# Second chunk's values one step sooner: a regrouped ScalarE and VectorE order for its last tiles, in top-k attention fused with two feed-forward layers

## The reference

```
scores = scale * q @ k.T                              # per batch and head, 576 x 576
kth    = 32nd largest of each row
attn   = softmax(where(scores >= kth, scores, -1e9))
x      = (attn @ v) as 2304 tokens x 512
x      = max(0.01 * h, h) @ w_out    with h = x @ w_in            # layer 0: 512 -> 2048 -> 512
out    = g @ w_out2                  with h = x @ w_in2           # layer 1
         g = h where h >= 1, 0 where h <= -1, (h + 1)^2 / 4 between
```

## Time and profile before

| | before |
|---|---|
| median of 3 runs | 1165.05 us (1163.45 to 1166.36) |
| time of the profiled execution | 1163.93 us |
| its span, first to last instruction | 1162.1 us |
| TensorE matmul busy | 1092.6 us, 94% |
| VectorE busy | 877.2 us, 75% |
| ScalarE busy | 791.6 us, 68% |
| GpSimd busy | 464.8 us, 40% |
| mean granted TensorE clock | 0.979 |

### The profile page before, as it was taken

How to read it: one execution, slowest core, us unless ns; L and a number is a source line. 1 busy time by engine, 2 the same in 40 slices (tenths; PEclk the granted TensorE clock), 3 DMA queues, 4 the chain that set the end, 5 groups by cost and what they waited for, 6 DMA issues and landing times.

```text
span 1162.1 us, 21227 instructions
## 1 busy us (share of the span) xinstructions
PE 1092.6 (94%) x7568; PEld 1002.3 (86%) x7568; DVE 877.2 (75%) x1921; ACT 791.6 (68%) x1827; POOL 464.8 (40%) x493
## 2 busy tenths in 40 slices
PE   5457998899999999999999999999999999999998
PEld 3336887799988998899999879989998999999998
DVE  7999999889889998999979989888993005300234
ACT  7887999787788877887869868778885224322332
POOL 5654468552264432643225434225532234222322
PEclk9679999999999999999999999999999999999999
DMA  7988988697657788788667667565555677787764
GB/s 247 351 337 298 366 307 311 217 377 252 234 201 237 246 307 289 274 291 293 237 232 245 220 218 247 203 211 192 169 195 210 213 257 253 254 285 251 256 246 139
DMA packets 90680, 295.52 MB, mean 254 GB/s; under 512 B 10064, under 2 KB 13776, under 8 KB 90576
## 3 DMA queue, kind: packets, MB, share of 16 engines
q1 hardware_dynamic: 86544, 289.45, 71.2%
q10 hardware_dynamic: 4032, 4.72, 1.1%
HBM read 255.85 MB, written 38.27 MB: 253 GB/s over the span
## 4 chain that ended last, share of the span: by engine, by line
PE 69%; DVE 18%; ACT 5%; issue 3%; POOL 3%; DMA 1%; SPq 0%; POOLq 0%; ACTq 0%; DVEq 0%
PE ps_f L928 19%; PE ps_f L936 18%; PE ps_f L929 18%; DVE top L1211 8%; DVE work L1215 7%; PE ps_av L887 6%; PE ps_s L848 3%; PE ps_t L864 2%; DVE part_r L1238 2%; PE ps_t L870 2%; DMA raw<-wd 1%; PE ps_t L848 1%; POOL gate L741 1%; ACT probs L1056 1%; ACT probs L1048 1%
## 5 line engine op out<-in xcount | busy, mean ns | idle before, releaser
L1211 DVE MAX8 top<-work 128x8 f32<-128x576 f32 x432 | 310.2, 743 | 0.2
L928 PE MATMUL ps_f<-xy,w_ring 128*128 128x384 f32 (+2 forms) x896 | 289.3, 323 | 5.7 <-ACT gate L1115 2.0
L928 PE MATMUL ps_f<-gate,w_ring 128*128 128x384 f32 (+2 forms) x896 | 285.2, 318 | 0.0
L936 PE MATMUL ps_f<-gate,w_ring 128*128 128x384 f32 (+2 forms) x896 | 280.9, 314 | 4.1 <-POOL gate L741 4.0
L936 PE MATMUL ps_f<-xy,w_ring 128*128 128x384 f32 (+2 forms) x896 | 281.1, 314 | 1.6 <-POOL xy L751 1.1
L929 PE MATMUL ps_f<-xy,w_ring 128*128 128x384 f32 (+2 forms) x896 | 280.3, 313 | 0.0
L929 PE MATMUL ps_f<-gate,w_ring 128*128 128x384 f32 (+2 forms) x896 | 279.8, 312 | 0.0
L1215 DVE MATCH_REPLACE8 work<-top,work 128x576 f32<-128x576 f32 x288 | 213.3, 740 | 0.0
L741 POOL TENSOR_TENSOR gate<-part_r,gate 128x384 fp32r<-128x384 f32 (+2 forms) x112 | 101.3, 905 | 244.0 <-ACT gate L1115 243.9
L928 PEld LDWEIGHTS ps_f<-xy,w_ring 128*128 128x128 f32 x896 | 169.7, 189 | 19.9 <-issue 10.1
L928 PEld LDWEIGHTS ps_f<-gate,w_ring 128*128 128x128 f32 x896 | 169.2, 189 | 6.5 <-issue 6.2
(11 more groups left out here) (85 smaller groups left out, 1842.0 us busy)
## 6 DMA issues: line engine op xcount, KB each, us to landing
w_ring<-w_split SPq DMA_DIRECT2D x408, 512.0 KB, 4.2
w_split<-w_ring SPq DMA_DIRECT2D x40, 512.0 KB, 6.3
raw<-wd SPq DMA_DIRECT2D x64, 256.0 KB, 5.8
w_split<-xy SPq DMA_DIRECT2D x24, 512.0 KB, 5.0
v_sb<-vd SPq DMA_DIRECT2D x32, 320.0 KB, 5.7
kq<-kqd SPq DMA_DIRECT2D x16, 480.0 KB, 4.9
kq<-kqd SPq DMA_DIRECT2D x15, 416.0 KB, 3.6
out_t<-y_acc ACTq DMA_DIRECT2D x12, 192.0 KB, 4.3
```

Source lines behind the costliest of these rows:

```text
L928: pe.matmul(out, w[:, 0, m], high, start=first, stop=False)
L936: mm = pe.matmul(out, w[:, 0, m], low, start=False, stop=end)
L1211: op = dve.max(top[:, t % TOP_SLOTS, 8 * r:8 * r + 8], source(t, r))
```

## The change

Four things change together.

1. `out_step` of items 18 and 19 is their last tile plus 5 instead of 6: they are transposed in steps 39 and 40, not in 40 and 41. Item 17 stays at 38. The values of gp 7 follow in step 40, not 41, so `READY[1]` is 41. The planner's `FIRST_FILL` becomes 3987 ns, and by its loop units 0 to 43 lie in steps 21 to 40, unit 44 is in step 41, and every later step holds what the step after it held, within one unit; units 248 to 335 are left for step 152. The order of the units is the same.
2. In steps 36 to 39, in which no ordinary tile has its exponential, the hurried tile (32 to 35) takes the ordinary place on ScalarE: `keep` ahead of the first group, `exponential` right behind it. Items 18 and 19 are normalised on ScalarE in their own step, behind the exponential, rather than in the step before.
3. VectorE's iteration 36 is written out: it ends tile 35 (third and fourth round) and then begins tile 36, closing item 18 in between.
4. Item 19's sum is closed in the middle of VectorE's iteration 37 rather than at its end.

```diff
+def sooner(it):
+    return hurried(it.gp) and it.gp == ITEM_OF[it.first - 1].gp
+
 def out_step(it):
-    return it.last + (5 if starts_early(it.gp) else 6 if hurried(it.gp) else 7)
+    return it.last + (5 if starts_early(it.gp) or sooner(it) else 6 if hurried(it.gp) else 7)
...
+SECOND_END = LAST_OF_GROUP[CHUNKS[1].last_gp]
...
                 done, t, soon = OUT_AT.get(s), exp_tile(s), hurried_tile(s)
+                if t is None and s >= READY[0]:
+                    t, soon = soon, None
...
                 if t is not None:
                     exponential(t)
-                if s + 1 in OUT_AT:
+                if done and sooner(done):
+                    normalise(done)
+                if s + 1 in OUT_AT and not sooner(OUT_AT[s + 1]):
                     normalise(OUT_AT[s + 1])
...
+            def finish_second(t, count, shut, first, second, third):
+                dve.wait_ge(dve_step, count)
+                top8(t - 1, 2)
+                for u in first:
+                    event(u)
+                dve.wait_ge(dve_step, count + 1)
+                drop8(t - 1, 2)
+                for u in second:
+                    event(u)
+                dve.wait_ge(dve_step, count + 2)
+                top8(t - 1, 3)
+                for u in third:
+                    event(u)
+                dve.wait_ge(scores_copied, 2 * ITEM_OF[t].n + 2)
+                top8(t, 0)
+                close_sum(shut)
+                dve.wait_ge(dve_step, count + 3)
+                drop8(t, 0)
+                dve.wait_ge(dve_step, count + 4)
+                invert_sum(shut)
+                if by_dve(shut):
+                    normalise(shut)
+                dve.wait_ge(dve_step, count + 5)
+                top8(t, 1)
+                dve.wait_ge(dve_step, count + 6)
+                drop8(t, 1)
...
-                early = shut is not None and starts_early(shut.gp)
+                early = shut is not None and (starts_early(shut.gp) or shut.last == SECOND_END)
...
+                if t == SECOND_END + 1:
+                    finish_second(t, count, shut, first, second, third)
                     count += 7
                     continue
```

More of the change, by code:

```diff
@@ L1277, in _ @@
                     finish_first(t, count)
+                    count += 7
+                    continue
+                if t == SECOND_END + 1:
+                    finish_second(t, count, shut, first, second, third)
                     count += 7
```

## The result

| | before | after |
|---|---|---|
| median, five runs each | 1164.2 us (1163.45 to 1166.36) | 1158.91 us (1158.24 to 1160.18) |
| ratio | | 0.9955, 95% interval 0.9944 to 0.9967 |
| span of the profiled execution | 1162.1 us | 1157.1 us |
| TensorE matmul busy | 1092.6 us | 1093.6 us |
| mean granted clock | 0.979 | 0.984 |

The kernel became 5.3 us faster; 5.5 was forecast. (The median before is of five runs here and of three in the table ahead of the prediction, 1165.05.) That the sum came so close is luck: two of its terms were wrong, by 2.0 and 2.8 us, and their errors nearly cancelled. The windows of the changed kernel, with the same columns as the earlier trace rows, show the stretch around the edit and what lies behind it.

A forecast was written before the change was run, and what follows sets the result against it. TensorE, busy 1092.6 of 1162.1 us, bounds the kernel, so only its waits and lower clock could move. Terms 1.7 + 1.5 + 1.3 + 1.4 - 0.4 = 5.5 us gave 1158.4, or 1159.5 against the median; range 1157 to 1161.5.

The forecast's parts named there:

- The gap ahead of gp 7's values: Step 40: TensorE waits about 1.2 us in all instead of 2.89; 1.7 us gained, between nothing and 2.9.
- its clock: Values of gp 7 run at full clock once the wait shrinks to pieces under a microsecond; 1.56 us gained, or nothing.
- Item 21's scores: Their wait for item 16's copy falls from 1.76 to about 0.5: 1.3 us gained, plus 1.37 from gp 6's clock.
- The shortest wait with a low clock: Around gp 6's and gp 7's values: 1.76 us is the shortest wait a low clock follows; shorter ones left open.
- The ScalarE-paced stretch: Steps in the thirties: waits of 1.8, 1.7 and 0.96 us stay; nothing gained, between 1.5 us more and 2 less.
- Later steps: Behind the edit: 15 scores or values products with little cover before, 16 after; 0.4 us lost.
- slower by the slip: Rival, steps 41 to 151: new pairings of units and items lose 10.3 us against 5.9 won, near 1169; chance 0.10.
- VectorE's order: Iteration 36: `finish_second` costs VectorE 0.6 us through waits between scans, hidden by its own 2.92 us wait; nothing.
- The clock falls all the same: Rival: waits shrink, but the clock still falls before gp 6's and gp 7's values; gain 2.6 us, 1162.5; chance 0.08.
- The waits only move: Rival: ScalarE's lag reappears at a bank or item 16's copy; gain 0 to 3.4 us, around 1163; chance 0.18.
- Everything is won: Rival: waits of the paced stretch shrink too; gain 8 to 11 us, around 1155; chance 0.08.
- The signs that I named: Profile after: gp 7's values some 5 us sooner, near 2.85 us; short waits; clock 1.00; later idle near 9.5 us.

The follow-up runs named there:

- first experiment: Kernel before, but in step 41 ScalarE copies item 19's transposition ahead of keep and exponential of tile 36; 1.0005, no gain.
- slip with the old orders: The change without ScalarE's swap for hurried tiles, without `finish_second` and without item 19's early close; 0.9947 against the kernel before.
- late slip: Kernel before, attention untouched, with one step's more units in step 52, all later steps following; 0.9977, 2.7 us faster than before.
- two-step slip: Kernel before with two steps' more units in step 52, all later steps following; 1.0 against the kernel before.
- plan of before: The change, but unit 44 may not begin before step 42, so every unit stands where it stood; 1.0049, 5.8 us slower than before.
- orders alone: The change with `sooner` always false, so steps and plan as before and only the new ScalarE and VectorE orders; 1.0003 against the kernel before.

## Why the prediction was right, and where it was not

**The gap ahead of gp 7's values** (1.7 us) **and its clock** (1.56 us): right. I had 1.2 us of waiting left; the profile has 0.46 and 0.38 ahead of the two transpositions, in the places named, and about 0.15 ahead of the values. The step's count, ScalarE against TensorE from the end of unit 41, was sound. But the cause is not the order on ScalarE alone, as I argued from the earlier trace rows. The first experiment removed just that and met GpSimd. I had written that GpSimd would have about a microsecond to spare because the splitting of kq moves behind it. In the changed kernel it has 0.43 us; GpSimd's timeline:

```profile
225.82 1.27 POOL L726 TENSOR_TENSOR w_ring<-raw,w_ring 128x512 fp32r<-128x512 f32 x1
227.52 0.88 POOL L738 TENSOR_TENSOR xy<-x_raw,xy 128x320 fp32r<-128x320 f32 x1 [0.43 <-ACT x_raw L1098]
```

In the first experiment GpSimd still had 1.06 us of kq's splitting to do ahead of that low half, at 223.35, which in the change stands behind it; that is half of the 2.2 us by which it was late (ScalarE's copy was there at 228.23, the low half began at 230.39). The spare is not what decides alone, however: the slip with the old orders has none, its TensorE waits 0.46 us for GpSimd, and it is as fast as the change. What the change and that kernel have in common is that items, units and the kq split move together.

**Item 21's scores** (1.3 us and 1.37 of clock): the mechanism held, the wait went to 1.08 rather than 0.5, so 0.7 us instead of 1.3. Of the clock see below. Over the stretch from unit 36 to 48 the ledger gives 5.4 us, where my four terms made 5.9.

**The shortest wait with a low clock** was misread. I wrote that 1.76 us is the shortest that a low clock follows in the kernel before. TensorE's timeline of that kernel, at gp 23's values, has waits of 0.49 and 1.41 us and then a slow 16 products, 3.73 us instead of 2.37:

```profile
678.90 0.41 PE L936 MATMUL ps_f<-gate,w_ring 128*128 128x320 f32 x1 [0.49 <-POOL gate L741]
...
681.01 0.42 PE L936 MATMUL ps_f<-gate,w_ring 128*128 128x320 f32 x1 [1.41 <-POOL gate L741]
...
682.40 3.73 PE L887 MATMUL ps_av<-p_t,v_sb 128*64 128x320 f32 x16
```

So the 1.08 us that item 21's scores still wait were nearer to such a fall than I had it, and that gp 6's values ran at full speed behind them (2.87 us) was less sure than the term says.

**The ScalarE-paced stretch** (nothing, between 1.5 more and 2 less): the term came out half a microsecond beyond its bad end. The losses between units 20 and 36 rose from 5.0 to 7.0 us. I counted that the same 12 units meet the same number of tiles, and did not look at what lies between the last output unit of layer 0 and the first unit of layer 1. Holding them apart did not help; the loss came back as waits for ScalarE's bank reads. That speaks for ScalarE's load over these steps as a whole, but which part of it costs the 2 us stays open.

**Later steps** (0.4 us lost): wrong in sign, and in kind. It was the term that the forecast missed most: 2.4 us gained from unit 48 on by the profiles, 2.7 us in the times of the late slip. Counting how many scores have little cover, 15 against 16, says nothing of their size. My reason for costing the slip at nothing, that TensorE is busy 640.51 of 650 us, was an argument about the last step and not about those 9.49 us of idle time, all of which the slip deals out anew. The rival "slower by the slip" had this mechanism and the wrong sign; the two-step slip, 2.7 us slower than the one-step one, shows that the sign is not to be had from the mechanism. Why this pairing is the better one stays open; the runs show only where it wins (4.4 us between units 48 and 170, 2.0 behind 230) and where it loses (4.0 between 170 and 230).

**VectorE's order** (nothing): right, and with `finish_second` left out the time is the same. The price of its waits was right too. VectorE's timeline of the changed kernel, in iteration 36:

```profile
205.49 0.76 DVE L1221 MAX8 top<-work 128x8 f32<-128x576 f32 x1
206.29 0.09 DVE L1225 MATCH_VALUE_LOAD work<-top,work 128x8 f32 x1
```

A scan that uses the one before it starts 0.80 us behind it, against 0.79 in the earlier trace rows. Scans with a scan between them and the one that they use start 0.66 us apart (203.12 and 203.78 in the kernel before), though they too wait for it. The Trainium skill ("VectorE: DVE Perf Modes", section "The DRAIN you can't avoid") has it, from a measurement of copies, that a semaphore costs nothing extra; for these scans the trace does not agree where the wait is for the scan just before, by 0.14 us each. It made no difference to the time.

**The load queues** (nothing): right, no wait for weights appears.

**The rivals.** "The clock falls all the same" did not happen in the changed kernel. "The waits only move" did not happen to the change, but to its first half made alone. "Everything is won" failed on the paced stretch.

**The signs that I named.** The clock of 1.00 from 203 to 232 us, the length of gp 7's values (2.84 us), the wait ahead of them, VectorE's wait in iteration 36 and the idle time behind (8.4 us of 650) came out as written, and none of the wrong signs appeared. Item 21's scores wait 1.08 us, where I had under 1. And the values of gp 7 begin only 1.0 us sooner (223.72 against 224.75), not some 5: by the ledger 0.8 us more went by up to unit 20 and 2.0 more up to unit 36, ahead of what was won.

## What to carry to other kernels

In a kernel whose engines walk one list of steps, moving one item by a step moves every later pairing; cost that as a term of its own with a range of both signs (here one step was worth 2.7 us and two steps nothing), and measure it alone by making the slip somewhere away from the edit. A wait removed on one engine is won only if the next engine in the hand-over was idle: read its timeline at the same microsecond, since here a wait made 1.6 us shorter on ScalarE came back as 2.3 us on GpSimd, and the lower clock with it. And when a part of a change is worthless alone, test it with its partner before giving it up: the sooner items without the sooner units were 5.8 us slower than before, with them 5.3 us faster.

## What the runs showed of the hardware

After the same wait in the same place the clock did not always do the same. Item 21's scores waited 1.76 us in the kernel before, in the first experiment and in both kernels with a late slip; the values behind them took 4.21, 4.53 and 4.55 us in the first three, and 2.87 in the two-step kernel, though all of these kernels are the same up to that point. The chain of work of the two-step kernel has:

```profile
202.17 2.87 PE ps_av L889 x20
224.35 4.61 PE ps_av L889 x20
```

A wait of 2.17 us at the same scores was followed by 3.82 us (the plan of before), one of 2.16 us by full speed (the orders alone). Gp 23 shows it once more: the waits of 0.49 and 1.41 us ahead of its values were followed by a granted clock of 0.50 in the kernel before, and the same waits, 0.50 and 1.42 us, by 1.00 in the plan of before, where the 16 products take 2.37 us. A wait of 2.9 us ahead of gp 7's values was followed by 4.4 to 4.6 us in all three profiles that have it; waits of 1.28, 1.33 and 2.07 by full speed, in the one profile that each had. So the 1.37 us that I booked for gp 6 are a matter of the execution as much as of the change.
